# Attention on TensorE: quarters of the array for the state read, a quarter of the scores left out, decay on the output

## The reference

```python
gamma = 1.0 - 2.0 ** (-5.0 - np.arange(H))
for t in range(S):
    state = gamma * state + einsum('bhd,bhe->bhde', k[:, :, t], v[:, :, t])
    y[:, :, t] = scale * einsum('bhd,bhde->bhe', q[:, :, t], state)
h = np.maximum(x @ w_in, 0.0);  x = h * h @ w_out
xn = x / rms(x) * rms_g
out = (silu(xn @ w_gate) * (xn @ w_val)) @ w_out2
```

## Time and profile before

| | |
|---|---|
| median of 3 runs | 1071.33 us |
| the profiled execution | 1070.97 us, its span 1069.2 us |
| PE, DVE, ACT, POOL busy, share of the span | 99%, 82%, 58%, 31% |
| granted TensorE clock over the span | 1.00 of full speed |
| attention on PE | from the first scores at 5.7 us to 89.6 us |

### The profile page before, as it was taken

How to read it: one execution, slowest core, us unless ns; L and a number is a source line. 1 busy time by engine, 2 the same in 40 slices (tenths; PEclk the granted TensorE clock), 3 DMA queues, 4 the chain that set the end, 5 groups by cost and what they waited for, 6 DMA issues and landing times.

```text
span 1069.2 us, 15711 instructions
## 1 busy us (share of the span) xinstructions
PE 1062.0 (99%) x5971; PEld 892.3 (83%) x5971; DVE 875.5 (82%) x939; ACT 622.0 (58%) x911; POOL 332.1 (31%) x242
## 2 busy tenths in 40 slices
PE   8999999999999999999999999999999999999998
PEld 7887888888888888888888888888888888888898
DVE  6696899878879878789799998978886986978684
ACT  3886775566765667664674645656444555444353
POOL 2754541004540005530035554005444102544000
PEclk9999999999999999999999999999999999999999
DMA  9999568763447644366642335632225751130455
GB/s 363 382 406 408 193 225 279 233 209 112 182 150 249 213 150 170 146 236 196 211 166 99 117 120 216 210 125 80 59 67 150 267 190 56 51 107 20 141 190 183
DMA packets 80586, 195.85 MB, mean 183 GB/s; under 512 B 24160, under 2 KB 34528, under 8 KB 75648
## 3 DMA queue, kind: packets, MB, share of 16 engines
q1 hardware_dynamic: 77872, 189.50, 51.1%
q10 hardware_dynamic: 2640, 5.36, 1.3%
HBM read 152.26 MB, written 42.48 MB: 182 GB/s over the span
## 4 chain that ended last, share of the span: by engine, by line
PE 95%; DMA 2%; ACT 1%; DVE 1%; SPq 0%; issue 0%; ACTq 0%
PE Y L841 13%; PE Y L842 13%; PE Y L843 13%; PE Z L841 9%; PE Z L843 9%; PE Z L842 9%; PE X L842 9%; PE X L841 9%; PE X L843 9%; DMA item_scratch<-ops 2%; PE Z L787 1%; PE Z L777 1%; PE Y L762 1%; PE R L807 1%; DMA qk_sb<-qkv 1%; PE X L762 1%
## 5 line engine op out<-in xcount | busy, mean ns | idle before, releaser
L686 POOL TENSOR_TENSOR w_ops<-raw_w,w_ops 128x512 fp32r<-128x512 f32 x90 | 127.9, 1421 | 491.4 <-ACT w_ops L969 491.2
L1029 ACT CAST ops<-hid 128x1024 fp32r<-128x1024 f32 x147 | 154.7, 1053 | 162.8 <-PE Z L843 55.1
L1412 DVE TENSOR_TENSOR ops<-hid,ops 128x1024 fp32r<-128x1024 f32 x147 | 180.1, 1227 | 45.4 <-ACT ops L1029 44.8
L686 POOL TENSOR_TENSOR w_ops<-sums_w,w_ops 128x512 fp32r<-128x512 f32 x120 | 167.6, 1399 | 125.5 <-ACT w_ops L969 125.0
L841 PE MATMUL Y<-ops,w_ops 128*128 128x512 f32 x360 | 140.2, 389 | 0.8 <-ACT u L1056 0.8
L842 PE MATMUL Y<-ops,w_ops 128*128 128x512 f32 x360 | 140.1, 389 | 0.0
L843 PE MATMUL Y<-ops,w_ops 128*128 128x512 f32 x360 | 140.1, 389 | 0.0
L1065 ACT ACTIVATE gt<-gt 128x512 f32<-128x512 f32 x72 | 45.1, 632 | 111.5 <-DVE gt L1629 38.9
L841 PE MATMUL Y<-ops 128*128 128x512 f32 (+1 forms) x288 | 104.4, 362 | 0.0
L842 PE MATMUL Y<-ops 128*128 128x512 f32 (+1 forms) x288 | 104.4, 362 | 0.0
L843 PE MATMUL Y<-ops 128*128 128x512 f32 (+1 forms) x288 | 104.4, 362 | 0.0
(11 more groups left out here) (176 smaller groups left out, 2344.9 us busy)
## 6 DMA issues: line engine op xcount, KB each, us to landing
ops<-item_scratch SPq DMA_DIRECT2D x147, 512.0 KB, 4.2
raw_w<-w_f SPq DMA_DIRECT2D x30, 1024.0 KB, 5.0
item_scratch<-hid SPq DMA_DIRECT2D x30, 512.0 KB, 3.1
qk_sb<-qkv SPq DMA_DIRECT2D x24, 512.0 KB, 8.0
kv_sb<-qkv SPq DMA_DIRECT2D x18, 512.0 KB, 8.4
y_scratch<-hid SPq DMA_DIRECT2D x12, 512.0 KB, 6.2
raw<-y_scratch SPq DMA_DIRECT2D x3, 2048.0 KB, 10.4
raw<-w_b SPq DMA_DIRECT2D x5, 1024.0 KB, 4.9
```

The lines of the kernel that those rows point to most:

```text
L686: nc.gpsimd.tensor_tensor(w_ops[:, k, 1], front_w_source(m, k), f32(w_ops[:, k, 0]), ALU.subtract).then_inc(w_lo, 1)
L1029: nc.scalar.copy(hop_at(n)[:, 0], hid[:, 2 * g:2 * g + 2, OPERAND[k], :]).then_inc(hop_hi, 1)
L1412: nc.vector.tensor_tensor(hop[:, 1], hid[:, 2 * g:2 * g + 2, OPERAND[k], :], f32(hop[:, 0]), ALU.subtract).then_inc(hop_lo, 1)
```

## The change

Four things change together in attention. The state read uses all four quarters of the array: an odd pair of heads writes its output to the other half of the columns (`y_rows`), and to the other bank of Z. The scores are made in pieces of 64 keys: the early 64 keys against all 128 queries, the late 64 keys against the last 64 queries only, so the quarter above the diagonal is left out (its place in PSUM is zeroed once at the start). The decay is no longer put on q before the state read, but on the output: VectorE multiplies by it as it copies the output out of Z (`copy_out`), and ScalarE no longer copies. The tables of mask and decay come ready from the host, so three matmuls and some copies of the start fall away. Both banks of Z now hold one chunk, so a chunk's read waits for the copy of the chunk before; the state has two places; the ring of q and k has 5 places; and a chunk's loads are all started by the end of the chunk five earlier.

```diff
-QKR, KVR = 4, 5
+QKR, KVR = 5, 5
+def y_rows(h):
+    half = (h + h // 2) % 2
+    return slice(D * half, D * half + D)
...
             for n in range(NCH - QKR):
-                b, c = divmod(n, CH)
-                sp.wait_ge(scores_done, n + 1)
-                if c:
-                    sp.wait_ge(q_scaled, (CH - 1) * b + c)
+                sp.wait_ge(chunk_done, n + 1)
+                if n == 0:
+                    sp.wait_ge(state_done, 1)
                 load_qk(n + QKR)
...
-                    load_kv(n + KVR - 1)
+                load_kv(n + KVR)
...
-                for h in range(H):
-                    rows = slice(D * (h % 2), D * (h % 2) + D)
-                    cols = slice(P * (h // 2), P * (h // 2) + P)
-                    mm = nc.tensor.matmul(scores_ps[n % 2][:, h % 2, cols], qk_sb[rows, n % QKR, KT, cols],
-                                          qk_sb[rows, n % QKR, QT, cols], start=True, stop=True)
+                for pairs, late in product(((0, 1), (2, 3)), range(2)):
+                    for p, f in product(pairs, range(2)):
+                        keys = D * ((p + late) % 2)
+                        rows, held = slice(D * f, D * f + D), slice(P * p + keys, P * p + keys + D)
+                        cols = slice(P * p + D * late, P * p + P)
+                        mm = nc.tensor.matmul(scores_ps[n % 2][keys:keys + D, f, cols], qk_sb[rows, n % QKR, KT, held],
+                                              qk_sb[rows, n % QKR, QT, cols], start=True, stop=True)
...
+            def y_place(h):
+
+                p = h // 2
+                return Z[y_rows(h), p % 2, P * (p // 2):P * (p // 2) + P]
...
                 if c:
                     pe.wait_ge(state_ready, (CH - 1) * b + c)
-                    pe.wait_ge(q_scaled, (CH - 1) * b + c)
+                if n:
+                    update(n)
+                    pe.wait_ge(y_copied, n)
+                if c:
                     for h in range(H):
                         p, rows = h // 2, head_rows(h)
-                        nc.tensor.matmul(y_ps[rows, p * P:(p + 1) * P], state[rows, p, :],
...
+                        nc.tensor.matmul(y_place(h), state[rows, c % 2, p, :], qk_sb[rows, n % QKR, QT, P * p:P * p + P],
+                                         start=p < 2, stop=False, skip_group_check=True)
...
             for n in range(NCH):
-                if 2 <= n + 1 < NCH:
-                    scale_k(n + 1)
-                copy_out(n)
+                if n + 2 < NCH:
+                    scale_k(n + 2)
+                store_x(n)
...
-            def scale_q(n):
+            def copy_out(n):
...
+                dve.wait_ge(chunk_done, n + 1)
...
+                    if 3 <= i and n < NCH - 1:
+                        dve.wait_ge(x_stored[i % 3], 16 * (i // 3))
+                    place = stored_y(n).rearrange("p (a b t) -> p a b t", a=2, b=2)
+                nc.vector.tensor_tensor(place.rearrange("p a b t -> p b a t"),
+                                        Z[:, :, 0:2 * P].rearrange("p b (a t) -> p b a t", a=2),
+                                        decay_y[:].rearrange("p b (a t) -> p b a t", a=2), ALU.mult)\
+                    .then_inc(y_copied, 1)
```

More of the change, by code:

```diff
@@ L444, in _ @@
             load_qk(0)
[L445 to L452, removed]
+            load_kv(0)
+            load_kv(1)
+            load_qk(3)
+            load_kv(2)
+            load_kv(3)
+            load_qk(4)
+            load_kv(4)
             for n in range(NCH - QKR):
-                b, c = divmod(n, CH)
-                sp.wait_ge(scores_done, n + 1)
-                if c:
-                    sp.wait_ge(q_scaled, (CH - 1) * b + c)
+                sp.wait_ge(chunk_done, n + 1)
+                if n == 0:
+                    sp.wait_ge(state_done, 1)
                 load_qk(n + QKR)
[L459 to L462, removed]
-                    load_kv(n + KVR - 1)
+                load_kv(n + KVR)
                 if n == 1:
@@ L782, in attend @@
                 pe.wait_ge(kv_loaded[n % KVR], 16 * (n // KVR) + 16)
                 pe.wait_ge(masked_ready, n + 1)
[L784 to L789, removed]
+                for h in (0, 1, 3, 2, 4, 5, 7, 6):
+                    p = h // 2
+                    mm = nc.tensor.matmul(y_place(h), kv_sb[:, n % KVR, V, h * D:(h + 1) * D],
+                                          masked[:, c % 2, h % 2, P * p:P * p + P],
+                                          start=c == 0 and p < 2, stop=True, skip_group_check=True)
@@ L810, in update, with zeros @@
                 mm.then_inc(state_done, 1)
[L812 to L820, removed]
-            pe.wait_ge(zeroed, 1)
[L823 to L828, removed]
+            def zeros(ps):
+                for f, p in product(range(2), range(PAIRS)):
+                    nc.tensor.matmul(ps[:, f, P * p:P * p + D], y_sb[:, 2, 0:P], y_sb[:, 2, 0:D], start=True, stop=True)
+            pe.wait_ge(zeroed, 1)
+            zeros(X)
+            zeros(Y)
             scores(0)
-            rows_times(decay_q_ps, 2).then_inc(decay_placed, 1)
-            zeros(3)
+            pe.wait_ge(rows_loaded, 16)
+            nc.tensor.matmul(R[:, 1, :], rows_sb[:, DM:], rows_sb[:, 0:DM], start=True, stop=True)\
+                .then_inc(decay_placed, 1)
             scores(1)
@@ L927, in _, with store_x @@
         def _(act):
-            def copy_out(n):
+            def store_x(n):
                 b, c = divmod(n, CH)
[L931 to L935, removed]
+                if (b, c) not in stored_chunks():
                     return
                 i = stored_chunks().index((b, c))
[L938 to L941, removed]
                 act.wait_ge(y_copied, n + 1)
-                act.dma_start(x_dram[i].rearrange("p h k t -> p (h k t)"), place)\
+                act.dma_start(x_dram[i].rearrange("p h k t -> p (h k t)"), stored_y(n))\
                     .then_inc(x_stored[i % 3], 16)
@@ L1813, in decay_tables @@
     h, t = np.arange(H)[:, None], np.arange(P)[None, :]
[L1814 to L1821 removed]
+    odd = (h // 2) % 2
+    token = np.where(odd, (t + D) % P, t)
+    place = [0, 2, 1, 3]
+    forward = [(scale * gamma[:, None] ** t) * (h // 2 == p) for p in place]
+    rows = np.concatenate(forward + [1.0 * (t // D == (h + odd) % 2)], axis=1)
+    causal = [1.0 * (t >= np.roll(np.arange(P), D * b)[:, None]) for b in range(2)]
+    back = (gamma[:, None] ** -token).T.reshape(P, PAIRS, 2).transpose(0, 2, 1)
     by_row = gamma.reshape(PAIRS, 2).repeat(D, axis=1).T
     s = by_row[:, None, :] ** (np.arange(CH)[None, :, None] * P - S // 2)
[L1824 to L1836 removed]
+    k = gamma[None, None, :] ** (S // 2 - P * np.arange(CH)[None, :, None] - token.T[:, None, :])
+    tables = np.concatenate([k.reshape(P, CH * H), s.reshape(P, CH * PAIRS)], axis=1)
+    factors = np.concatenate([back.reshape(P, H)] + causal, axis=1)
+    return [np.ascontiguousarray(a.astype(np.float32)) for a in (rows, factors, tables)]
 def kernel(q, k, v, moe_w_in, moe_w_out, moe2_w_gate, moe2_w_val, moe2_w_out, moe2_rms_g):
```

129 lines of the change are left out of this document (57 added, 72 removed).

## The result

The change makes the kernel slower: 1082.98 us median of four runs (1080.99 to 1084.19) against 1071.12 on the same chip, ratio 1.0109, 95% interval 1.0092 to 1.0127. The profiled execution took 1080.99 us with a span of 1079.2; against the 1070.97 of before that is 10.0 us more. The other three took 1.7 to 3.2 us longer than this one, at granted clocks of 0.995 to 0.997 where it has 0.998; what follows is read from the profiled one. The prediction was 1067.6.

The account below looks back on a forecast made before the run. TensorE, busy 99%, was taken as the bound; its work shrinks 13.2 us, but stores of items let only 3.7 through: 1070.97 - 3.7 = 1067.3, median 0.36 above, 1067.6. Range 1065.0 to 1071.2.

Parts of the forecast that it names:

- The array: TensorE in attention: four quarters run side by side, a middle chunk takes 3.04 in place of 3.60, sum -13.2 us.
- The slow rival: TensorE in attention: quarters don't run four at a time, a middle chunk takes 4.14, +10.0 us, 1081.3; 14%.
- The third: Rival on attention's scores: they stay at 1.09, 6.5 us less won, 1069.2; no own chance, inside first rival and forecast.
- my DMA paragraph: Loads and stores: same bytes, a faster TensorE fills the hole at 41 to 57 us, transfers come 2.0 us earlier.
- The start: Zeroing matmuls, first scores, 512-wide matmul, second scores: between -1.6 and +0.1 us, taken as 0.
- VectorE: Attention, chunks 11 to 20: VectorE needs 34.1 us against TensorE's former 33.0, sets the pace, about 3.4 us a chunk.
- the forecast 84.5: End of attention: 5.1 us earlier than 89.62 after VectorE's stretch, so near 84.5.
- DMA and the items: Behind attention: stores of items 0 and 1 decide, ScalarE free at 89.4, fifth product at 98.3 not 102.00, 3.7 us won.
- The wait that I forecast: Behind attention: ScalarE's last two casts wait for stores of items 0 and 1, and the rest of TensorE's 13.2 becomes waiting.
- the first rival: VectorE and DMA hold all: win 1.7, or 0.6 with attention ending at 89; 1069.7 to 1070.7, taken as 1070; 25%.

Follow-up runs that it names:

- experiments 9 to 11: Changed kernel with whole scores and later decay matmul, 1072.1 us; start, loads and VectorE's order mended too, 1070.9; that with scores in quarters, 1082.47. The last two are the pair.
- tiny loads: Changed kernel, but from the sixth chunk on each load of q, k and v brings 64 of its 512 columns: 1071.85 us.
- experiment 12: Changed kernel with loads of 64 columns from the sixth chunk on and the 512-wide decay matmul moved behind the first chunk: 1073.3 us.
- the best one: Changed kernel with scores in eight matmuls, later decay matmul, mended start, VectorE moving first state before first output, one load started earlier: 1070.9 us, ratio 0.9995.
- whole scores with the later decay matmul: Changed kernel with scores in eight matmuls of 128 keys again and the 512-wide decay matmul behind the first chunk: 1072.1 us, ratio 1.001.
- experiment 8: Changed kernel with rings of 4 places for q, k and for k, v in place of 5: 1082.93 us.
- experiment 2: Changed kernel, but from the sixth chunk on each load of q, k and v brings only the first 64 of its 128 partitions: 1081.65 us.

## Why the prediction was wrong

**The array: right.** Scores 0.83 (0.82 forecast), read 0.60 (0.59), update 0.62 (0.61), V 1.02, together 3.07 against 3.04. Four quarters run at once; their first instructions start within 0.02 us in the records. The slow rival, whose 1081.3 lies near the result, gave it for a reason that isn't there: no chunk takes over 3.60 for its array. The third, scores no shorter, is out with the 0.83.

**The step that failed** is the first: "time is won only where TensorE's own work gets shorter, and only if what it meets next is ready". I looked for what it meets among engines, places and loads, and took the instructions themselves as there. I priced the scores' sixteen matmuls in place of eight by slots of the array and never by their number. Missing term: some 10 us of attention (99.51 against 89.46 with the gaps, the slow clock behind them and waits for loads gone); its core is time in which TensorE waits for instructions, 9.3 us after the change, and 12.9 against none in the pair of experiments 9 to 11. The other half of it was my DMA paragraph, which counted a nearly full DMA as a matter of when loads and stores land; instructions wait longer then, too (4.1 us, 0.0 to 1.7 with tiny loads).

**The start, taken as 0: wrong by 3.4 to 3.8 us.** The zeroing went as I priced it, 0.22 us each, to 8.1 us. Behind it I put scores at 0.82 and the 512-wide matmul at 0.87, and V as later, as if TensorE ran at its later pace; they took 1.49, 2.07 and 1.90, and pace makes 2.6 us of the loss. The rest is that I let the 512-wide matmul follow the first scores at once: it stands ahead of the second scores, and its 20 KB of decay rows, fourth in ScalarE's queue, land 0.6 us too late. The first update starts at 15.69 after and 15.28 with tiny loads, against 11.91.

**VectorE: right in kind, and close in size.** Without gaps its chunks 11 to 20 come every 3.4 us, as forecast (chain of waits with tiny loads, starts of the output's copy):

```profile
53.83 0.61 DVE y_sb L1304
...
57.28 0.42 DVE y_sb L1304
...
60.20 0.68 DVE y_sb L1304
...
63.72 0.58 DVE y_sb L1304
...
67.24 0.68 DVE y_sb L1304
```

Attention then ends 5.0 us behind the forecast 84.5. Its first update is 3.4 us late, which would leave 1.6; but that the start's loss reaches the end of attention is not shown, as experiment 12, which should have shown it, ended later.

**DMA and the items: not reached in the changed kernel, nor in the best one.** In both the fifth product is no closer to the end of attention than before. The wait that I forecast does exist: in the run of whole scores with the later decay matmul ScalarE's last two casts wait for the stores of items 0 and 1, the second until 93.39, and the fifth product comes at 102.80, 13.5 us behind the end of attention at 89.33 (timeline of ScalarE):

```profile
91.66 0.62 ACT L1000 CAST spare<-raw_w 128x512 fp32r<-128x512 f32 x1 [8.16 <-DMA item_scratch<-spare]
93.39 0.62 ACT L1000 CAST spare<-sums_w 128x512 fp32r<-128x512 f32 x1 [1.10 <-DMA item_scratch<-spare]
```

But no version with all its loads brought the transfers 2 us forward: these two stores land 3 us later than before in this run, and 1 us later in the best one. In the best version VectorE holds attention near the 89 of the first rival, which was taken as 1070; it measured 1070.9. This version has the longer scores; whether quarters with their instructions in time would have passed it no run shows, since the one with tiny loads moves far fewer bytes ahead of the stores.

**Could it be read beforehand?** The danger could, the size only in part. The trace before has the transfers of instructions, and between the entry into a block and the use of the next 5.1 us of the 7.1 that a block lasted. 256 instructions at the forecast 3.04 us for 160 are 4.9. By the mean that lacks 0.2 us a block; by the longest waits before, 3.8 us, it lacks 1.3. That the wait would grow from 2.7 to 4.1 us in the mean was not to be read, and what makes it grow stays open: the ring of q and k has a place more and the loads are asked for differently, but experiment 8 doesn't settle it.

## What to carry to other kernels

When a change cuts work into more and smaller instructions, count instructions per us, weight loads with them, not only the array's columns, and compare the time of 256 of them with the time in which the next 256 arrive while DMA is full; here 26 to 28 ns an instruction left no gap or one of 0.55 us, and 19 to 20 left ten. A gap in a busy engine for which the profile names no releaser, at equal counts of instructions, points to this; it is told apart by thinning the transfers, or by splitting instructions in the kernel that has no gaps.

## What was not expected of the hardware

Halving a load to 64 of 128 partitions didn't relieve the DMA engines: a 4 KB packet took 0.28 us in place of 0.16 (medians, 20 to 80 us), with 15 under way at a time in place of 16. And a gap of 2 us in TensorE can cost more than its own length: after the one at 84.76 the granted clock showed 0.89 in that stretch and 0.94 in the next, 1.5 us more. It need not: behind a gap of 2.2 us at 46.94 in experiment 2 no fall stands (1.00 from 48 to 52 us).
